# Attention that feeds a routed mixture of experts: the end flag read one double later and written after the slots, SyncE out of a barrier, the experts' first double in halves, and the first v load in five pieces with the queue held behind it

## The chip, the cores and the metric

The kernel runs on one core of a Trainium2 chip. The metric is the device time of one execution in microseconds (us). The engines are called as in the profile: PE is TensorE (matmuls), PEld its weight loads, DVE is VectorE, ACT is ScalarE, POOL is GpSimd, SP is SyncE. A `q` behind a name (PEldq, SPq) marks what that engine's sequencer does itself: register work, waits, branches, and the issue of DMAs.

## The reference

```python
scores = (1 / S) * z @ z.T              # 8 batches, S = 3072, z has 64 columns
attn   = maximum(scores, 0) ** 2
x      = (u * (attn @ v)).reshape(24576, 256)

logits = x @ w_gate                     # 8 experts, each token goes to its largest logit
gate_w = softmax probability of that expert
for i in range(24576):                  # in order: a token gets the next slot of its expert
    keep[i] = counts[e] < capacity      # capacity 768: later tokens of a full expert are dropped
h   = maximum(disp[e] @ w1[e], 0)       # 768 x 256 by 256 x 1024
y   = h @ w2[e]
out[i] = gate_w[i] * y[e, pos[i]]       # 0 for a dropped token
```

Tokens are placed in order, so once all eight experts are full no later token changes the output.

## The kernel before

The attention works through groups of 384 queries, eight groups to a batch, numbered n; g is n & 7. Group 0 is written out ahead of the loop ("peeled"). A group has twelve doubles c = 0..11, each of two chunks of 128 keys: four matmuls make scores into PSUM `Sc` (`scores`, L607 and L608), ACT applies Relu in place (L432) and squares into `attn` (L436), DVE splits the square into two fp16 parts (`attn_hi` L907, `attn_lo` L913), and 18 matmuls weigh v with them into `O` (`weigh`, L642, L644, L646). Scores run LEAD = 3 doubles ahead of the weighing; z and v are split into fp16 halves too (`first_z`, `v_hi`, `v_lo`), by scales from their maximum and their absolute sums (`v_sum`, L408, then DVE L925, a POOL reduction, three DVE steps).

At the end of group n-1 DVE multiplies `O` by u (`gate_x`, L952 and L956). During group n these rows are scaled and split (DVE L1005 writes the last part), SP transposes them by three DMAs (L259, `xT`), PE makes the logits at double 3 (L682), DVE picks the expert (L1041 to L1051), PE counts tokens (L690 to L697), and DVE works out the slots (L1067 to L1079). POOL scatters the rows to `disp` in HBM by three indirect DMAs (L350). In the same chain DVE writes a word to `ends` (L1074): 0 if all experts are full, NG + 1 otherwise. Every engine reads it in each group, after double END_AT (`load_end`, called by `both_parts`): it waits on `flag_ready`, loads the word into a register (L224), and branches. On 0, PE closes its accumulations (`close`, L708), issues filler matmuls that nobody reads (`turn_over`, L614), and leaves. The scores of double c + LEAD and their waits on the keys stand in the program ahead of the weighing of c; the matmuls for the norms of the next batch (`next_norms`, g = 3 alone) stand behind a branch at the end of double 6.

SP's part in group 0: load z and v of batch 0, `wg`, `ubuf`; fill the 6144 rows of `disp` with an empty row (eight DMAs from one SBUF row, L287); load z and v of batch 1 (L273, L278); wait until these have all landed (L216); and only then start on group 1, which begins with the three transposes. All of it is one queue, in program order. POOL waits for the fill (`disp_filled`) before it lets DVE overwrite rows.

The experts follow: five engines meet at `attention_over`, SP waits for PE (`pe_over`) and for the scatters, then loads dispatched rows by a transposing DMA and their tail (factor and token) by a plain one (`load_rows`, L315, L317). Per block of 384 rows there are four doubles of the hidden layer: 12 matmuls (`hidden`, L755), ACT Relu to fp16 (`high`, L541), DVE the rest (`low`, L1207). `hidden` of double q waits for `low` of double q - 2, since they share PSUM. DVE's factors come from the tails (`row_factors`, L1202).

## Time and profile before

| what | value |
|---|---|
| median of 3 runs | 886.45 us (885.63 to 886.87) |
| profiled execution, its own time | 889.07 us |
| its span | 887.3 us |
| PE busy, share of the span | 867.8 us, 98% |
| DVE, ACT, POOL busy | 71%, 64%, 14% |
| granted TensorE clock, mean | 0.996 |

The profiled execution took 2.6 us more than the median; the span is 1.8 us shorter than its own time. Busy time of PE counts pipelined matmuls whose ends are modelled, so a start-to-start distance says more of its pace than the busy share: 0.11 us for a matmul with 256 columns, 0.16 us for one with 384, at the full clock. The scored part of the loop ends at about 621 us, in group 18.

### The profile page before, as it was taken

Reading aid. Unit: us, or ns where it says so; the run is one execution under the profiler, and the core shown is the slowest. Engines: PE = TensorE matmul, PEld = TensorE weight load, DVE = VectorE, ACT = ScalarE, POOL = GpSimd, SP = SyncE. Lnnn points to the kernel's source line nnn. Section 1 sums busy time; section 2 is a strip of 40 time slices with the busy share of each in tenths; the row PEclk is TensorE's granted clock in tenths of the full one; section 3 lists DMA queues with packets and bytes.
Section 4 is the critical chain, followed back from the end, with each engine's and each line's share of the span. In section 5 each row is a group of like instructions: output and inputs, shape, how many; then the busy total and the mean of one; then the engine's idle time right before and its main releaser. Section 6 shows DMA issues by size and latency. Waiting matters only on the chain.

```text
span 887.3 us, 22840 instructions
## 1 busy us (share of the span) xinstructions
PE 867.8 (98%) x7397; PEld 690.7 (78%) x7398; DVE 630.9 (71%) x1346; ACT 572.1 (64%) x871; POOL 120.2 (14%) x119
## 2 busy tenths in 40 slices
PE   5999999999999999999999999999899999999997
PEld 4877787887788888888888888888677777777776
DVE  6976867888888888788888887677255565655531
ACT  6968776768768669787777876777144344434422
POOL 0001102101101101110110110110112112121212
PEclk8999999999999999999999999999999999999999
DMA  9955619624633650110111012411714245225100
GB/s 287 205 190 179 195 36 348 195 57 139 195 89 107 232 178 20 51 41 24 42 53 25 28 51 55 168 42 35 166 42 150 54 130 166 84 94 154 51 20 35
DMA packets 105991, 97.87 MB, mean 110 GB/s; under 512 B 63869, under 2 KB 94666, under 8 KB 104816
## 3 DMA queue, kind: packets, MB, share of 16 engines
q1 hardware_dynamic: 101072, 84.92, 32.9%
q0 software_dynamic: 4896, 12.64, 4.0%
q8 instruction: 14, 0.23, 0.1%
q14 instruction: 9, 0.07, 0.0%
HBM read 40.03 MB, written 44.93 MB: 96 GB/s over the span
## 4 chain that ended last, share of the span: by engine, by line
PE 91%; DMA 3%; issue 2%; ACT 1%; SPq 1%; DVE 1%; POOL 0%; ACTq 0%; POOLq 0%; DVEq 0%
PE O L642 16%; PE O L646 15%; PE O L644 15%; PE Sc L755 14%; PE Sc L607 8%; PE Sc L608 8%; PE O L776 3%; PE O L778 3%; PE O L780 3%; DMA rawv<-in_v 2%; PE M L778 2%; PE M L776 2%; PE M L780 2%; ACT Sc L432 1%; PE M L682 1%
## 5 line engine op out<-in xcount | busy, mean ns | idle before, releaser
L646 PE MATMUL O<-vS,attn_lo 128*128 128x256 f16 x1332 | 363.0, 273 | 0.0
L642 PE MATMUL O<-vS,attn_hi 128*128 128x256 f16 x1332 | 363.0, 273 | 0.0
L644 PE MATMUL O<-vS,attn_hi 128*128 128x256 f16 x1332 | 363.0, 273 | 0.0
L913 DVE TENSOR_TENSOR attn_lo<-attn,attn_hi 128x768 f16<-128x768 f32 x224 | 214.7, 958 | 7.7
L432 ACT ACTIVATE Sc<-Sc 128x768 f32<-128x768 f32 x224 | 178.2, 795 | 51.7 <-PE Sc L608 41.3
L436 ACT ACTIVATE attn<-Sc 128x768 f32<-128x768 f32 x224 | 181.7, 811 | 7.1
L607 PE MATMUL Sc<-zP 128*128 (+1 forms) x450 | 147.3, 328 | 7.0 <-ACT attn L436 5.3
L642 PEld LDWEIGHTS O<-vS,attn_hi 128*128 128x128 f16 x1332 | 130.3, 98 | 27.6 <-DVE ubuf L952 1.0
L644 PEld LDWEIGHTS O<-vS,attn_hi 128*128 128x128 f16 x1332 | 130.3, 98 | 26.5
L907 DVE CAST attn_hi<-attn 128x768 f16<-128x768 f32 x224 | 125.3, 560 | 34.1 <-ACT attn L436 30.3
L608 PE MATMUL Sc<-zQ,zP 128*128 (+1 forms) x450 | 147.0, 327 | 0.0
L1207 DVE SCALAR_TENSOR_TENSOR rawv<-Sc,rawv 128x768 f16<-128x768 f32 x64 | 61.1, 956 | 113.9 <-ACT rawv L541 113.9
L646 PEld LDWEIGHTS O<-vS,attn_lo 128*128 128x128 f16 x1332 | 130.3, 98 | 15.1
L350 POOL DMA_INDIRECT disp<-xrow,slot x54 | 68.6, 1270 | 480.3 <-DVE slot L1078 444.3
L541 ACT ACTIVATE rawv<-Sc 128x768 f16<-128x768 f32 x64 | 51.9, 811 | 114.5 <-PE Sc L755 113.2
L755 PE MATMUL Sc<-vS,w1h 128*128 128x384 f16 x512 | 104.1, 326 | 2.0 <-DVE rawv L1207 1.6
L755 PEld LDWEIGHTS Sc<-vS,w1h 128*128 128x128 f16 x512 | 49.9, 98 | 30.5 <-ACT rawv L541 1.9
L776 PE MATMUL O<-w2s,rawv 128*128 128x256 f16 x256 | 69.8, 273 | 0.0
L780 PE MATMUL O<-w2s,rawv 128*128 128x256 f16 x256 | 69.8, 273 | 0.0
L778 PE MATMUL O<-w2s,rawv 128*128 128x256 f16 x256 | 69.8, 273 | 0.0
L607 PEld LDWEIGHTS Sc<-zP 128*128 128x128 f16 (+1 forms) x450 | 44.0, 98 | 31.4 <-ACT attn L436 9.6
L385 POOL DMA_INDIRECT out<-attn,vS x48 | 46.9, 977 | 123.5 <-ACT attn L553 109.7
(147 smaller groups left out, 891.1 us busy)
## 6 DMA issues: line engine op xcount, KB each, us to landing
out<-empty SPq DMA_DIRECT2D x8, 3072.0 KB, 11.7
wraw<-in_moe_w SPq DMA_DIRECT2D x16, 1024.0 KB, 7.7
rawv<-in_v SPq DMA_DIRECT2D x12, 768.0 KB, 11.6
ubuf<-in_u SPq DMA_DIRECT2D x19, 384.0 KB, 3.2
disp<-empty SPq DMA_DIRECT2D x8, 774.0 KB, 17.8
rawz<-in_z SPq DMA_DIRECT2D x3, 768.0 KB, 6.3
rawv<-in_v SPq DMA_DIRECT2D x1, 1024.0 KB, 7.5
rawv<-in_v SPq DMA_DIRECT2D x1, 896.0 KB, 9.2
```

What stands on the lines that cost most here:

```text
L432: act.activation(pair, pair, ACT.Relu).then_inc(s["relu_done"], 1)
L436: act.activation(attn[:, c % BUFS, :, :], Sp[:, 2 * (c % 2):2 * (c % 2) + 2, 0:GROUP], ACT.Square, scale=ROOT_C).then_inc(s["square_done"], 1)
L607: nc.tensor.matmul(to, keys, zP[:, bass.ds(qb, GROUP)], start=True, stop=False)
L608: ins = nc.tensor.matmul(to, keys, zQ[:, bass.ds(qb, GROUP)], start=False, stop=True)
L642: nc.tensor.matmul(o_part(t), hi, v[:, 0:D], start=c == 0 and j == 0 and t % 2 == 0, stop=False, skip_group_check=True)
L644: nc.tensor.matmul(o_part(t), hi, v[:, D:2 * D], start=False, stop=False, skip_group_check=True)
L646: ins = nc.tensor.matmul(o_part(t), lo, v[:, 0:D], start=False, stop=c == PAIRS - 1 and j == 1, skip_group_check=True)
L755: ins = nc.tensor.matmul(Sp[:, 2 * (p % 2) + fi, 0:GROUP], w[par][:, m, f * P:(f + 1) * P], xt[:, k, x + m, :], start=(at == 0), stop=(at ...
L776: nc.tensor.matmul(y_part(t), hi, w2s[:, par, f, 0:D], start=f == 0, stop=False, skip_group_check=True)
L778: nc.tensor.matmul(y_part(t), hi, w2s[:, par, f, D:2 * D], start=False, stop=False, skip_group_check=True)
L907: dve.tensor_copy(attn_hi[:, b, :, :].rearrange("p j n -> p (j n)"), attn[:, b, :, :].rearrange("p j n -> p (j n)")).then_inc(s["hi_done"], 1)
L913: dve.tensor_tensor(attn_lo[:, b, :, :], attn[:, b, :, :], attn_hi[:, b, :, :], ALU.subtract).then_inc(s["lo_done"], 1)
```

## The change

Four parts, with fillers set anew around them. (1) END_AT goes from 5 to 6, and DVE computes the slots first and the flag behind them, with two more waits of its own steps. (2) SP no longer counts in `attention_over`: 3 instead of 4. (3) The first double of the experts: PE signals after the first of its two halves (`h_first`), ACT and DVE handle it in two halves, and DVE does the first two doubles ahead of the two `row_factors`. (4) v of batch 0 comes in pieces of 4, 6, 6, 5, 3 chunks instead of 8, 7, 5, 4, and SP waits for the last piece before it issues `wg` and all behind it. Fillers: 40 to 56 and 20 to 28 at the beginning, 72 to 44 after `close`, 56 to 36 after the barrier. In group 0 the scores of double 3 stand behind the weighing of double 0.

```diff
@@ SP, group 0
-            for q, name in enumerate("abcd"):
+            for q, name in enumerate("abcde"):
                 sp.dma_start(rawv[:, V0_PIECES[q]:V0_PIECES[q + 1], :], v[0, :, V0_PIECES[q]:V0_PIECES[q + 1], :]
                              ).then_inc(s["loaded_v0" + name], 16)
+            sp.wait_ge(s["loaded_v0e"], 16)
             sp.dma_start(wg[:, :, :], w_gate).then_inc(s["loaded_wg"], 16)
...
             attention_loop(sp, body)
-            sp.sem_inc(s["attention_over"], 1)
             sp.wait_ge(s["pe_over"], 1)
@@ ACT, experts
-            high(0, 0)
+            act.wait_ge(s["h_first"], 1)
+            act.activation(hh[:, 0, 0, :], Sp[:, 0, 0:GROUP], ACT.Relu).then_inc(s["hh_first"], 1)
+            act.wait_ge(s["h_ready"], 1)
+            act.activation(hh[:, 0, 1, :], Sp[:, 1, 0:GROUP], ACT.Relu).then_inc(s["hh_done"], 1)
             high(1, 1)
@@ PE
             scores(1, 0, 1, 0)
-            turn_over(40)
+            turn_over(56)
             scores(2, 0, 2, 0)
-            turn_over(20)
+            turn_over(28)
...
-                            scores(K0 + c + LEAD, n, c + LEAD, par)
+                            if not peeled or c:
+                                scores(K0 + c + LEAD, n, c + LEAD, par)
...
+                        if peeled and c == 0:
+                            scores(K0 + LEAD, n, LEAD, par)
...
-                    turn_over(72)
+                    turn_over(44)
...
-            pe.wait_ge(s["attention_over"], 4)
-            turn_over(56)
+            pe.wait_ge(s["attention_over"], 3)
+            turn_over(36)
...
+                    if isinstance(q, int) and q == 0 and fi == 0:
+                        ins.then_inc(s["h_first"], 1)
@@ DVE, slots
-                            dve.tensor_tensor(base[:, 1, :], base[:, 0, :], M[1][:, 32:32 + E], ALU.add)
                             route(dve.tensor_tensor(posf[:, :, :], counts, over_tiles(base[:, 0, :]), ALU.add))
-                            dve.tensor_tensor(over[:, :], base[:, 1, :], limit[:, :], ALU.subtract)
+                            dve.tensor_tensor(base[:, 1, :], base[:, 0, :], M[1][:, 32:32 + E], ALU.add)
                             route(dve.tensor_tensor(fullp[:, :, :], posf[:, :, :], over_tiles(limit[:, :]), ALU.is_ge))
-                            dve.tensor_reduce(least[:, :], over[:, :], AX.X, ALU.min)
                             route(dve.scalar_tensor_tensor(out=posf[:, :, :], in0=fullp[:, :, :], scalar=float(FAR // 2),
                                                            in1=posf[:, :, :], op0=ALU.mult, op1=ALU.add))
+                            route(dve.tensor_tensor(posf[:, :, :], posf[:, :, :], onehot[:, :, :], ALU.mult))
+                            dve.tensor_reduce(slot[:, :], posf[:, :, :], AX.X, ALU.max).then_inc(s["slot_ready"], 1)
+                            route(dve.tensor_tensor(over[:, :], base[:, 1, :], limit[:, :], ALU.subtract))
+                            route(dve.tensor_reduce(least[:, :], over[:, :], AX.X, ALU.min))
                             dve.tensor_scalar(ends[0:1, bass.ds((n - 1) & (NG - 1), 1)], least[0:1, :],
                                               0.0, float(NG + 1), ALU.is_lt, ALU.mult
                                               ).then_inc(s["flag_ready"], 1)
-                            route(dve.tensor_tensor(posf[:, :, :], posf[:, :, :], onehot[:, :, :], ALU.mult))
-                            dve.tensor_reduce(slot[:, :], posf[:, :, :], AX.X, ALU.max).then_inc(s["slot_ready"], 1)
@@ DVE, experts
+            for fi, done in enumerate(("hh_first", "hh_done")):
+                dve.wait_ge(s[done], 1)
+                ins = dve.scalar_tensor_tensor(out=hl[:, 0, fi, :], in0=Sp[:, fi, 0:GROUP], scalar=0.0,
+                                               in1=hh[:, 0, fi, :], op0=ALU.max, op1=ALU.subtract)
+            ins.then_inc(s["hl_done"], 1)
+            low(1, 1)
             row_factors(0, 0)
             row_factors(0, 1)
-            low(0, 0)
-            low(1, 1)
@@ constants
-V0_PIECES = (0, 8, 15, 20, 24)
+V0_PIECES = (0, 4, 10, 16, 21, 24)
-END_AT = 5
+END_AT = 6
```

Three places show what this does to the order on an engine. The first is SP's queue from its third row on, at the beginning of the program, before the change (`rawv` is v, `disp<-empty` the fill, the last two rows the load of batch 1).

```order
L242 DMA rawv<-in_v 128x2048
L242 DMA rawv<-in_v 128x1792
L242 DMA rawv<-in_v 128x1280
L242 DMA rawv<-in_v 128x1024
L244 DMA wg<-in_moe_w_gate 128x16
L260 DMA ubuf<-in_u 128x768
L287 DMA disp<-empty 128x6x258 [waits empty_ready]
L287 DMA disp<-empty 128x6x258 x7
L273 DMA rawz<-in_z 128x1536 [waits klo_ready,khi_ready]
```

The same stretch with the change; the fill, 6.2 MB, now stands behind a wait on v.

```order
L242 DMA rawv<-in_v 128x1024
L242 DMA rawv<-in_v 128x1536 x2
L242 DMA rawv<-in_v 128x1280
L242 DMA rawv<-in_v 128x768
L245 DMA wg<-in_moe_w_gate 128x16 [waits loaded_v0e]
L261 DMA ubuf<-in_u 128x768
L288 DMA disp<-empty 128x6x258 [waits empty_ready]
L288 DMA disp<-empty 128x6x258 x7
L274 DMA rawz<-in_z 128x1536 [waits klo_ready,khi_ready]
```

What moved is `wg`, `ubuf` and everything after them: they can't be issued before v has landed.

The second place is PE's read of the flag inside the loop, before the change: it stands between the last matmul of double 5 and the scores issued in double 6, which carry waits on the keys.

```order
L646 MATMUL O<-vS,attn_lo 128x256
L224 REGISTER_ALU [waits flag_ready]
L224 REGISTER_ALU
L224 ISA
L224 TENSOR_LOAD ends
L207 COMPARE_AND_BRANCH
L198 REGISTER_ALU x2
L601 REGISTER_ALU [waits khi_ready,klo_ready]
L607 MATMUL Sc<-zP 128x384 [waits square_done]
```

With the change it stands one double further down, behind the branch for the norms (its four matmuls are skipped unless g is 3).

```order
L207 REGISTER_ALU
L207 COMPARE_AND_BRANCH
L585 MATMUL M<-zsq,onesb 128x384 [waits norm_step]
L585 MATMUL M<-zsq,onesb 128x384 x3
L207 UNCONDITIONAL_BRANCH
L224 REGISTER_ALU [waits flag_ready]
L224 REGISTER_ALU
L224 ISA
L224 TENSOR_LOAD ends
L207 COMPARE_AND_BRANCH
L604 REGISTER_ALU
L610 MATMUL Sc<-zP 128x384 [waits square_done]
```

The key waits are no longer behind the read, and the norms' branch is now ahead of it.

The third place is DVE's tail of the slot chain with the change (before it, the flag's three instructions stood among those of the slots, as the diff shows).

```order
L1080 TENSOR_TENSOR posf<-posf,onehot 128x24
L978 REGISTER_ALU
L1081 TENSOR_REDUCE slot<-posf 128x3
L1082 TENSOR_TENSOR over<-base,limit 128x8
L978 REGISTER_ALU
L1083 TENSOR_REDUCE least<-over 128x1
L978 REGISTER_ALU
L1084 REGISTER_ALU
L1084 ISA
L1084 TENSOR_SCALAR ends<-least 1x1
L1087 COPY base<-base 128x8
L914 REGISTER_ALU
```

The slot is written before the flag is begun, and the next cast of `attn` stands behind both.

## Rows read from the trace of the kernel before

**Rows 1.** Who waited for whom, whole span: us in total, times, longest.
```profile
PE Sc L607 <- ACT attn L436: 5.3, 2, 5.0
...
DVE ends L1074 <- DVE posf L1072: 4.0, 18, 0.2
...
PE Sc L755 <- DVE rawv L1207: 1.6, 1, 1.6
...
PE M L682 <- DMA xT<-xrow: 0.6, 1, 0.6
```

**Rows 2.** Timeline of the beginning: start, us, engine line operation, idle before.
```profile
17.04 1.06 ACT L408 ACTIVATE vS<-rawv 128x1024 f16<-128x1024 f32 x1 [2.38 <-DMA rawv<-in_v]
...
18.22 0.80 ACT L432 ACTIVATE Sc<-Sc 128x768 f32<-128x768 f32 x1
...
19.91 0.50 PE L607 MATMUL Sc<-zP 128*128 128x384 f16 x1 [5.02 <-ACT attn L436]
...
21.36 1.01 DVE L896 SCALAR_TENSOR_TENSOR vS<-rawv,vscale,vS 128x768 f16<-128x768 f32 x1
...
24.35 0.27 PE L642 MATMUL O<-vS,attn_hi 128*128 128x256 f16 x1
```

**Rows 3.** Stretches: length; PE, PEld, DVE, ACT, POOL busy; PEclk, DMA share, GB/s.
```profile
0.00:14.00 14.00, 9.42 (x93) 8.12 (x95) 9.32 (x65) 7.68 (x10) 0.21 (x5) 1.00 0.86 315
...
16.00:18.00 2.00, 0.00 (x0) 0.00 (x0) 0.00 (x0) 0.96 (x1) 0.00 (x0) 0.82 1.15 217
...
20.00:24.00 4.00, 4.00 (x27) 2.99 (x28) 3.93 (x6) 3.94 (x6) 0.00 (x0) 0.50 1.10 218
...
44.00:52.00 8.00, 8.00 (x70) 6.60 (x68) 5.75 (x12) 4.97 (x7) 0.36 (x1) 1.00 1.01 382
```

**Rows 4.** Line L216, SP's sequencer behind its wait for batch 1: ns; start.
```profile
L216 SPq MOVE  x1: 29/29/29, 56.8 to 56.8; - x1
```

**Rows 5.** The critical chain from group 1's first transpose to its logits: start, us, what.
```profile
59.97 1.31 SPq L259
...
63.79 2.42 DMA xT<-xrow
...
66.35 0.45 PE M L682 x12
```

**Rows 6.** Loads of the flag (L224), groups 1 to 7, then 8 to 18: ns min/median/max, starts.
```profile
L224 PEldq TENSOR_LOAD <-ends x7: 895/932/1203, 70.8 to 266.0; - x7
...
L224 PEldq TENSOR_LOAD <-ends x11: 302/306/320, 298.6 to 619.7; - x11
```

**Rows 7.** PE's sequencer around the read in group 2, by line: ns; first and last start.
```profile
L200 PEldq EVENT_SEMAPHORE  x3: 51/51/51, 102.9 to 105.0; - x3
...
L198 PEldq ALU_OP  x2: 36/36/36, 104.6 to 104.7; - x2
...
L601 PEldq ALU_OP  x2: 32/32/32, 101.0 to 105.1; - x2
...
L207 PEldq ALU_OP  x1: 36/36/36, 105.9 to 105.9; - x1
L207 PEldq COMPARE_BRANCH  x1: 213/213/213, 106.0 to 106.0; - x1
```

**Rows 8.** Timeline, the gap on PE behind that read.
```profile
104.76 0.27 PE L646 MATMUL O<-vS,attn_lo 128*128 128x256 f16 x1
105.22 0.33 PE L607 MATMUL Sc<-zP 128*128 x1 [0.19 <-issue]
```

**Rows 9.** Timeline around the end of the attention loop.
```profile
621.55 4.18 PE L614 MATMUL O<-ones,identh 128*128 128x128 f16 x72
626.27 3.30 PE L614 MATMUL O<-ones,identh 128*128 128x128 f16 x56 [0.54 <-SPq L310]
```

**Rows 10.** Timeline of the experts' first doubles.
```profile
634.58 1.81 DVE L1207 SCALAR_TENSOR_TENSOR rawv<-Sc,rawv 128x768 f16<-128x768 f32 x2
...
635.67 0.81 PE L755 MATMUL Sc<-vS,w1h 128*128 128x384 f16 x4 [1.56 <-DVE rawv L1207]
```

More of the change, by code:

```diff
@@ L177, in y_part @@
             return (Oa[:, 0, 0:D], Mp[:, 0, 0:D], Oa[:, 1, 0:D])[t]
-        names = """consts empty_ready loaded_z00 loaded_z01 loaded_wg loaded_v0a loaded_v0b loaded_v0c loaded_v0d
+        names = """consts empty_ready loaded_z00 loaded_z01 loaded_wg loaded_v0a loaded_v0b loaded_v0c loaded_v0d loaded_v0e
             zsq0 v_high vparts0 vsum0 nrm0 mx0 amx0 scales0 vsum_done nrm_psum nrm_done zhi_ready khi_ready zlo_ready klo_ready loaded_zv loaded_u loaded_w0 loaded_w1
@@ L189, in relu2_attention_moe @@
             h_ready hh_done hl_done y_summed y_ready y_scattered0 y_scattered1 y_scattered2
-            y_scattered3 fac_ready"""
+            y_scattered3 fac_ready h_first hh_first"""
         s = {n: sem(n) for n in names.split()}
@@ L409, in v_sum @@
                                       ACT.Abs, scale=1.0 / SUM_SCALE, accum_out=vsum[:, bass.ds(column, 1)])
-            for q in range(SLICES):
-                act.wait_ge(s["loaded_v0" + "abcd"[q]], 16)
+            for q in range(len(V0_PIECES) - 1):
+                act.wait_ge(s["loaded_v0" + "abcde"[q]], 16)
                 v_sum(q, V0_PIECES[q], V0_PIECES[q + 1] - V0_PIECES[q]).then_inc(s["vparts0"], 1)
@@ L536, in _ @@
             act.sem_inc(s["y_ready"], TILES)
-            act.wait_ge(s["attention_over"], 4)
+            act.wait_ge(s["attention_over"], 3)
             def high(q, p):
@@ L923, in _ @@
             first_z(2)
-            dve.wait_ge(s["vparts0"], SLICES)
-            dve.tensor_reduce(mx[:, 1:2], vsum[:, 0:SLICES], AX.X, ALU.add).then_inc(s["vsum0"], 1)
+            dve.wait_ge(s["vparts0"], len(V0_PIECES) - 1)
+            dve.tensor_reduce(mx[:, 1:2], vsum[:, 0:len(V0_PIECES) - 1], AX.X, ALU.add).then_inc(s["vsum0"], 1)
             dve.wait_ge(s["amx0"], 1)
@@ L1066, in over_tiles @@
                                 return x.unsqueeze(1).to_broadcast([P, TILES, E])
+                            route(dve.tensor_tensor(posf[:, :, :], counts, over_tiles(base[:, 0, :]), ALU.add))
                             dve.tensor_tensor(base[:, 1, :], base[:, 0, :], M[1][:, 32:32 + E], ALU.add)
-                            route(dve.tensor_tensor(posf[:, :, :], counts, over_tiles(base[:, 0, :]), ALU.add))
-                            dve.tensor_tensor(over[:, :], base[:, 1, :], limit[:, :], ALU.subtract)
                             route(dve.tensor_tensor(fullp[:, :, :], posf[:, :, :], over_tiles(limit[:, :]), ALU.is_ge))
-                            dve.tensor_reduce(least[:, :], over[:, :], AX.X, ALU.min)
                             route(dve.scalar_tensor_tensor(out=posf[:, :, :], in0=fullp[:, :, :], scalar=float(FAR // 2),
                                                            in1=posf[:, :, :], op0=ALU.mult, op1=ALU.add))
+                            route(dve.tensor_tensor(posf[:, :, :], posf[:, :, :], onehot[:, :, :], ALU.mult))
+                            dve.tensor_reduce(slot[:, :], posf[:, :, :], AX.X, ALU.max).then_inc(s["slot_ready"], 1)
+                            route(dve.tensor_tensor(over[:, :], base[:, 1, :], limit[:, :], ALU.subtract))
+                            route(dve.tensor_reduce(least[:, :], over[:, :], AX.X, ALU.min))
                             dve.tensor_scalar(ends[0:1, bass.ds((n - 1) & (NG - 1), 1)], least[0:1, :],
@@ L1196, in _ @@
             dve.drain().then_inc(s["attention_over"], 1)
-            dve.wait_ge(s["attention_over"], 4)
+            dve.wait_ge(s["attention_over"], 3)
             def row_factors(i, k):
@@ L1268 @@
 VLO_AT = (7, 8)
-ROUTE_STEPS = 2 + 2 + 2 + 4 + 3
+ROUTE_STEPS = 2 + 2 + 2 + 3 + 6
 _INS = ['u', 'v', 'z', 'moe_w_gate', 'moe_w1', 'moe_w2']
```

## The prediction, as put on record before the changed kernel ran

> **What bounds the kernel now.** I read four views: who waited for whom over the span, the timeline of the beginning, the critical chain, and the timeline around the end of the attention loop. PE is the engine that sets the end. It is busy 98% of the span, and nearly all its waits after its start stand in five places. In the waits view the reader is to see how short that list is: 5.0 us once at the beginning, where PE waits for ACT's first squares; 1.6 us once in the experts; 0.6 us once for a transpose [rows 1]; 0.5 us once for SP [rows 9]. A fifth kind is small and repeated, a gap where PE's sequencer issued nothing in time: in group 2 the last matmul of double 5 starts at 104.76 and the next at 105.22, 0.46 apart where 0.11 is due, so 0.35 us are lost [rows 8]. So an edit is worth what it takes from these places, less what it makes late elsewhere. The profiled execution took 889.07 us, 2.6 more than the median of 886.45; all terms are differences within the trace, and I take them over to the median unchanged. About 0.2%, 1.8 us, is what a measurement of this kernel can tell from no change.
>
> **1. The flag read, six gaps of 0.35 us and one larger.** The sequencer reaches the wait for the flag at 102.9 and the first scores behind it start at 105.22, so its path is 2.3 us long [rows 7, 8]. It runs ahead of the array by what is queued: the last queued matmul gives out at 104.87, 1.95 us after 102.92. The longest piece of the path is the load of the flag, 0.93 us in groups 1 to 7, 0.31 later [rows 6]; at 0.31 the path is 1.7 and fits in 1.95, so the gap is a matter of groups 1 to 7. With the change the pieces from the first L198 at 104.6 to L601 at 105.1 (key waits, 0.5 us) fall out of the path, and the norms' branch comes ahead of the wait: L207 at 105.9, then a branch of 0.213 from 106.0, some 0.37 in all [rows 7]. The path becomes 2.3 - 0.5 + 0.37 = 2.15, the gap 0.2 instead of 0.35: 0.15 in each of six groups, and about 0.25 in group 1, where the load took 1.2. Sum -1.2 us. Bounds: 0, if the branch and the load cost more behind the norms, and 6 x 0.35 + 0.7 = -2.8, if no gap is left. I take -1.2, worked out from the pieces. That the flag is written a little later (behind the slots) costs nothing: the read moves by a whole double, 2.6 us. DVE's cast behind the slots is delayed by two waits of its own steps, some 0.2 us each as the flag's wait now [rows 1], under the 2.6 us of a double by which the splits run ahead of PE.
>
> **2. The end of the loop, one double more.** The double adds 4 x 0.16 + 18 x 0.11 = 2.6 us on PE and 28 fillers of 0.058 fall away, -1.6. The fillers ended at 621.55 + 4.18 = 625.73, and SP let PE go on at 626.2, so SP was last by 0.5 [rows 9]. Now PE's drain comes at 625.73 + 1.0 = 626.7, and SP, which waits for it too, is ready before: the slots lose the flag's instructions ahead of them, whose last alone made DVE wait 0.2, 18 times [rows 1]. The rows of the experts are asked for 0.5 later. That SP is out of the barrier is therefore worth nothing: PE frees itself, but the rows set the start. +0.5 us; bounds 0 (drain earlier than modelled) and +1.0.
>
> **3. The first double in halves.** PE stood idle for 1.56 us until 635.67, when DVE's first `low` came in, which started only at 634.58 behind two factor steps that wait for tails [rows 10]. With `low` ahead of them and halves of 0.45 to 0.55 us on ACT and DVE, the first double is split at about 3 us after PE starts, PE needs 3.9 for its two doubles, and the wait is gone: -1.7, the idle 1.56 and the tail of a matmul that the idle time leaves out. Bounds: -1.7 and -1.0, the latter, if the second double's `low`, queued behind on DVE and needed 3.9 later, or the row loads come into it.
>
> **4. The beginning.** Two things happen. First, v lands earlier. ACT waited 2.38 us for the last piece, until 17.04, so it could have started at 14.66 [rows 2]; the landing is between these, and I take 15.6, the middle, since nothing but v is then in the queue. ACT then has 3 chunks instead of 4 (-0.2), so Relu starts 1.3 before its 18.22. PE's first weighing needs the first split of v, which ended at 22.37; it started at 24.35 for want of PE [rows 2]. At the full clock PE would be there at 21.1, and the moved scores (0.65) follow: a gain G of 24.35 - 21.1 - 0.65 = 2.6 us. At half clock, which was granted from 17.3 (0.82 of 2 us from 16 on) to 24 in and after PE's idle 5 us [rows 3], scores and 28 fillers take 1.3 + 3.0 us from 18.6, so 22.9 and G = 0.3 to 0.8. Fillers of 56 leave 2.8 us of idle, not 5, so both are open. Either way PE is up to 2.6 us early in group 0.
>
> Second, the fill of `disp` starts later, and group 1 hangs on it. Before, 14 us at 315 GB/s moved 4.4 MB [rows 3]; z, v, `wg` and `ubuf` are 4.3 MB, so the fill began by 13.9. Now `wg` is issued at 15.6, `ubuf` at 16.1, the fill at 16.6; with 1.1 us to the first byte, as for z at the start, and 1.1 us for `ubuf`, the fill flows from 18.35. That is 4.45 us later. The DMA share is 1.0 or more from there to 52, at 217 GB/s in the fill and 382 in batch 1 [rows 3], so nothing absorbs the delay. SP's wait for batch 1 ended at 56.8, three microseconds before the rows of group 1 were there to be transposed at 59.97, so it cost nothing [rows 4, 5]. It now ends at 56.8 + (3.9 to 4.6) = 60.7 to 61.4, and the transposes start 0.3 later, at 61.0 to 61.7 instead of 59.97. From the first issue to the last landing they took 6.24 us (59.97 to 63.79 + 2.42) [rows 5]; back to back, two issues of 1.31 and the last one's 2.42 are 5.0 at least. The logits, at 66.35 before, come at 66.1 to 68.0. PE would have been there at 65.5 - G. So the gain of the beginning is waited away in group 1, and this term is 0 to +1.6; I take +0.5. What hid the fill was ACT's and DVE's work in group 0; what is late next is `xT`. Past it, everything on PE follows the logits as before.
>
> Against this the Trainium skill speaks (DMA: Bandwidth & Descriptors, Rules for kernel authors and Specifications): issue a DMA early and wait late, and the fabric carries up to 435 GB/s with rows above 512 bytes at line rate. The first half is against the new wait. By the second, an estimate, the fill of 6.2 MB would take 14 us and batch 1 would be in long before 57, and term 4 would be -G. The rows of the fill are 1032 bytes and ran at half that rate, so the sum goes by the trace.
>
> **Sum.** -1.2 + 0.5 - 1.7 + 0.5 = -1.9 us: 884.5.
>
> **Rivals.**
> A, the forecast: the terms above, 883.2 to 886.0.
> B, the queue is in time: the fill catches up, or L216 ends by 59, and PE keeps G. For it: ACT's 2.38 us wait for the last piece of v, while the fill is already flowing at the same time [rows 2, 3], says that some part of the DMA engines runs behind the others; if the end of batch 1 is theirs too, they lose less by the hold than the others do. Against it: a DMA share over 1.0, that is no slack in the mean. Then -2.4 - (1.0 to 2.6) = 881.4 to 883.0.
> C, slower than before: PE waits 2.5 to 3.5 us at the logits of group 1, and the clock is halved for it, as it was after 5.0 us of idle and was not after 1.6 in the experts [rows 1, 3]: the mean clock of 0.996 leaves room for one half-clock stretch of 7 us in the span, and that is the one at the beginning. A stretch at half clock is 6.7 us long in the trace (17.3 to 24) and loses half of that, 3.4: 884.5 + 3.4 = 887.9, and 889 if v lands as late as before (+1.4). It decides from a wait of some 2.5 us on, so it needs both a G near 2.6 and the late fill. The Trainium skill (TensorE: Matmul & The Clock Gate, Part 1) has the throttled clock as the default that activity lifts, which the trace bears out at the start; it gives no other time here.
> D, the read does not gain: term 1 is 0, since the branch for the norms takes what the key waits give. 885.7.
>
> **How the numbers follow.** A 0.47, B 0.25, C 0.20, D 0.08. Below 884.7 lie B and about half of A: faster 0.50. Within 0.2% lie the rest of A, D and half of C: 0.40. Slower 0.10. The range takes in B down to 881.8 and C up to 887.8.
>
> **What would show it.** Term 1: the gap behind L224's load in groups 2 to 7 at 0.2, no L198 between load and scores. Term 2: PE's drain near 626.7, less what came before, and SP's first expert load right behind it. Term 3: no wait of L755 for `rawv`. Term 4: SPq L216 at 60.7 or later instead of 56.8; L682 waiting for `xT` 1.5 to 4 us; first weighing at 21 or 22.9. Wrong if L216 stays near 57 to 58 (B), or if PEclk shows 0.5 in group 1 (C).

## The result, and the profile after

The changed kernel took 892.34 us (median of 4 runs, 891.41 to 893.28) against 886.12 us (4 runs) for the kernel before: ratio 1.0065, interval 1.005 to 1.008. It is slower; 884.5 was forecast, with 887.8 as the upper end. The profiled execution took 893.28 us with a span of 891.5.

First, who waited on PE over the whole span (total, times, longest), the view of [rows 1]:

```profile
PE M L686 <- DMA xT<-xrow: 5.9, 2, 5.0
...
PE Sc L610 <- ACT attn L436: 3.6, 4, 1.2
PE Sc L761 <- DMA vS<-disp: 1.3, 1, 1.3
```

The wait for ACT's first squares (5.0 in [rows 1]) is short now, and the wait for DVE's `low` in the experts is gone. In their place PE waits 5.0 us, once, for the transposed rows `xT` ahead of the logits of group 1. The stretches around it (length; PE, PEld, DVE, ACT, POOL busy; PEclk, DMA share, GB/s) and the logits themselves, as in [rows 3, 5]:

```profile
62.00:67.60 5.60, 0.61 (x15) 0.36 (x14) 0.00 (x0) 0.00 (x0) 0.00 (x0) 1.00 0.42 81
67.70:71.00 3.30, 3.30 (x17) 2.01 (x15) 1.80 (x11) 2.29 (x4) 0.00 (x0) 0.50 0.91 319
71.10:76.00 4.90, 4.90 (x48) 4.01 (x47) 3.89 (x14) 3.40 (x6) 1.91 (x2) 1.00 1.03 349
...
67.30 0.45 PE L686 MATMUL M<-wgs,xT 128*128 128x16 f16 x12 [4.99 <-DMA xT<-xrow]
```

All engines stand still for it, and the 3.3 us behind it run at half clock: 1.7 us lost. SP's wait for batch 1, the fill of `disp` and the batch's first load show why, against 56.8 in [rows 4]:

```profile
15.61 19.41 SPq L288 DMA_DIRECT2D disp<-empty  x8
35.13 4.67 SPq L274 DMA_DIRECT2D rawz<-in_z  x1
...
L216 SPq MOVE  x1: 29/29/29, 61.4 to 61.4; - x1
```

The beginning of PE did what was hoped, and more (compare [rows 2]; at 24.35 before):

```profile
16.95 0.34 PE L610 MATMUL Sc<-zP 128*128 128x384 f16 x1 [1.16 <-ACT attn L436]
...
19.66 0.27 PE L645 MATMUL O<-vS,attn_hi 128*128 128x256 f16 x1 [0.33 <-DVE vS L904]
```

Behind group 1 the changed kernel loses more. In groups 2, 9 and 10 there is a wait for ACT's square in the second half of the group (start, us, idle time before), where [rows 1] had one such wait beside that of the beginning, 0.3 us in group 9:

```profile
120.92 0.27 PE L649 MATMUL O<-vS,attn_lo 128*128 128x256 f16 x1
121.91 0.33 PE L610 MATMUL Sc<-zP 128*128 x1 [0.72 <-ACT attn L436]
...
350.08 0.33 PE L610 MATMUL Sc<-zP 128*128 x1 [1.11 <-ACT attn L436]
...
381.95 0.27 PE L649 MATMUL O<-vS,attn_lo 128*128 128x256 f16 x1
382.87 0.33 PE L610 MATMUL Sc<-zP 128*128 x1 [0.64 <-ACT attn L436]
```

A yardstick for the loop is the time from group 1's logits to group 18's. These are the last ones, before and after, with the first hidden matmul of the experts behind them (the starts are what counts here; of the logits' twelve matmuls the rows hold only those in the stretch that was asked for):

```profile
615.40 0.25 PE L682 MATMUL M<-wgs,xT 128*128 128x16 f16 x4
630.04 0.82 PE L755 MATMUL Sc<-vS,w1h 128*128 128x384 f16 x4 [0.47 <-DMA vS<-disp]
```

```profile
620.88 0.17 PE L686 MATMUL M<-wgs,xT 128*128 128x16 f16 x1
...
635.96 0.82 PE L761 MATMUL Sc<-vS,w1h 128*128 128x384 f16 x4 [1.27 <-DMA vS<-disp]
```

So the loop takes 615.40 - 66.35 = 549.05 us before and 620.88 - 67.30 = 553.58 after, of which 1.7 is the half clock; the loop's end takes 14.64 and 15.08.

### The profile page after: what moved, and what is told of

Same layout as the page of the kernel before. It is cut to its first block, busy times and chain, and to the rows that moved or that the text cites. A ratio compares the mean times of both kernels' runs of the same rounds, so it can differ in the third digit from the quotient of the medians.

```text
span 891.5 us, 22911 instructions
## 1 busy us (share of the span) xinstructions
PE 868.9 (97%) x7395; PEld 690.5 (77%) x7396; DVE 634.7 (71%) x1349; ACT 573.8 (64%) x878; POOL 114.4 (13%) x119
## 4 chain that ended last, share of the span: by engine, by line
PE 80%; DVE 6%; issue 5%; ACT 3%; DMA 3%; ACTq 1%; SPq 1%; PEld 1%; DVEq 0%; POOL 0%; PEldq 0%; POOLq 0%
PE Sc L761 14%; PE O L645 13%; PE O L647 13%; PE O L649 13%; PE Sc L610 7%; PE Sc L611 6%; PE O L784 3%; PE O L786 3%; PE O L788 3%; DMA rawv<-in_v 2%; ACT Sc L432 2%; PE M L786 2%; PE M L784 2%; PE M L788 2%; DVE attn_hi L915 1%
## 5 line engine op out<-in xcount | busy, mean ns | idle before, releaser
L432 ACT ACTIVATE Sc<-Sc 128x768 f32<-128x768 f32 x225 | 179.1, 796 | 55.6 <-PE Sc L611 46.5
L350 POOL DMA_INDIRECT disp<-xrow,slot x54 | 62.4, 1156 | 490.0 <-DVE slot L1081 449.5
```

The lines of the kernel that those rows point to most:

```text
L432: act.activation(pair, pair, ACT.Relu).then_inc(s["relu_done"], 1)
```

## The experiments

Four series on four chips; each comparison is with the kernel before on the same chip, in the same series. "Loop" below is the yardstick just named, read from each run's own trace.

### What the hold costs: no_hold

```diff
-            sp.wait_ge(s["loaded_v0e"], 16)
             sp.dma_start(wg[:, :, :], w_gate)...
```

> The changed kernel without SP's wait for the last piece of v; all else stays. Theory (the hold makes batch 1 late, PE waits 5 us for xT in group 1 and is then granted half the clock for 3.4 us): L216 ends near 57, the wait for xT in group 1 falls under 1 us, PEclk stays at 1.00 from 62 to 76, and all groups from group 2 on start 2.6 us earlier than in the changed kernel: 889.7 us, and down to 888.5 if PE also keeps part of what it gained in group 0. Rival (the half clock in group 1 comes from the longer fillers and the moved scores, not from the wait): PEclk still falls in group 1 and the time stays at 891 or more. Second rival (v lands later again without the hold and eats what is won): the first weighing starts at 24 instead of 19.7, but since group 1's logits set the pace, 889.7 stays.

886.44 us, ratio 1.0002 (0.9992 to 1.0012). L216 ended at 52.9, and group 1's logits waited for nothing of note:

```profile
61.71 0.45 PE L685 MATMUL M<-wgs,xT 128*128 128x16 f16 x12
```

The clock stays at 1.00, and the first weighing is at 19.9 without the hold too, so the second rival is out, and so is the first. The time came out 2 to 3 us under the 888.5 to 889.7 that were expected: the expectation went from 892.3, and what a slow fill does to the changed kernel is not in this series (see after_again). The forecast's B, an early group 1, is what this edit gives. But the loop takes 551.99, so 2.9 us are still lost in it, and v needs no hold to come early.

### ACT's read: act_read and both

Behind double 6 ACT first reads the flag, then sums v; `both` has no hold either.

```diff
                 def part(start, stop):
+                    if start and not peeled:
+                        extras(END_AT)
                     for c in range(start, stop):
...
-                        if not peeled and (c in VHI_AT or c in ZHI_AT):
+                        if not peeled and c != END_AT:
+                            extras(c)
```

> The changed kernel, with ACT's reading of the flag moved ahead of its own extra work of double 6 (the sum of v and the wait for it in groups 1, 2, 9, 10, 17 and 18); the hold of the fill stays. Theory (ACT's read is exposed behind the sum of v, where ACT's queue has been emptied, and costs 0.3 to 0.8 us each in groups 2, 9, 10 and 17): the gaps on PE of 0.88 in group 2, 1.27 in group 9, 0.80 in group 10 and 0.31 in group 17 go back to the 0.2 to 0.45 of their neighbours, and the time falls by 2 to 2.6: 890.0 us. Rival (those groups are late because DVE writes the flag and the slots later, or because of PE's own read): the gaps stay, 892.3. The 2.6 us of group 1 stay in both.

> The changed kernel without the hold and with ACT's read of the flag ahead of its extra work. Theory: the two costs are separate and add up, 892.3 - 2.6 - 2.3 = 887.4 us; what is left against the kernel before are the double more at the loop's end (+0.4), the halves in the experts (-1.7), PE's shorter gap behind the read (-0.7) and some 0.9 to 1.5 of groups 8 and 9 that neither names; without those, 884.5. Rival (they hide each other: with one gone, the other's delay is what remains): within 1 us of the better one of the two single edits.

act_read 886.98 (1.0014, 1.0003 to 1.0025), both 885.99 (0.9997, 0.9986 to 1.0008). The first number looks like a triumph of the theory (892.3 to 890.0 was expected) and is none: the time came from group 1, which this edit doesn't touch, and where the logits came at 62.73 instead of 67.30. Group 10 of the changed kernel, and then of act_read, on ACT:

```profile
370.26 0.19 ACT L408 ACTIVATION_READ_ACCUMULATOR xT<-rawv  x1
371.59 0.80 ACT L432 ACTIVATE Sc<-Sc 128x768 f32<-128x768 f32 x1 [1.14 <-issue]
372.42 0.81 ACT L436 ACTIVATE attn<-Sc 128x768 f32<-128x768 f32 x1
...
375.36 0.81 ACT L436 ACTIVATE attn<-Sc 128x768 f32<-128x768 f32 x1
```

```profile
363.42 0.84 ACT L408 ACTIVATE xT<-rawv 128x768 f16 x1 [0.80 <-issue]
364.17 0.19 ACT L408 ACTIVATION_READ_ACCUMULATOR xT<-rawv  x1
364.70 0.80 ACT L432 ACTIVATE Sc<-Sc 128x768 f32<-128x768 f32 x1 [0.34 <-ACT xT L408]
...
375.98 0.33 PE L616 MATMUL Sc<-zP 128*128 x1 [0.53 <-ACT attn L436]
```

1.14 us of idle behind the sum became 0.80 ahead of it and 0.34 behind it: the same. PE's wait in group 10 stayed (0.53 against 0.64), in group 2 (0.72) and in group 9 (1.01 against 1.11) as well. The edit moved the cost, it did not take it away, and couldn't tell the theory from its rival. `both` shows the same: loop 551.75 against 551.99 without the edit, 0.2 us, and a time within 0.5 us of no_hold's, as the rival had it.

### The changed kernel again, and the hold alone: after_again, hold_only

hold_only is the kernel before with one line more:

```diff
+            sp.wait_ge(s["loaded_v0d"], 16)
             sp.dma_start(wg[:, :, :], w_gate)...
```

> The changed kernel once more, with a profile, in one series with the others. In its first profile the fill of disp was issued from 15.6 on, batch 1 was in at 61.5 and PE waited 5.0 us for xT; with ACT's read moved (which should not touch group 1 at all) the fill was issued at 15.1, batch 1 was in at 56.9 and the wait was 0.9. Theory (the hold leaves batch 1 without slack, and the rate at which the fill and the batch run, which differs from execution to execution, then decides over 4 to 5 us): the time spreads over 886.5 to 893 over series, and the profile's wait for xT goes with the end of L216, 1.0 + (L216's end - 57) us. Rival (the moved read did it): 892 and a wait of 5.0 us again.

> The kernel before, with SP waiting for the last piece of v ahead of wg, ubuf and the fill, and nothing else. Theory (the hold brings v in earlier but batch 1 later): the first weighing at 21 to 22, L216's end 3 to 4 us later than the 53.9 to 56.8 seen without a hold, the logits of group 1 from 1 us earlier to 2 us later than before, 885.7 to 888.5; I put 886.7. Rival (the fill catches up, the hold costs nothing and v's gain stays): 884.

The changed kernel took 888.06 here, ratio 1.0028 (1.0016 to 1.004), not 1.0065. In its trace the fill, the batch and the logits:

```profile
15.02 16.97 SPq L288 DMA_DIRECT2D disp<-empty  x8
32.09 3.90 SPq L274 DMA_DIRECT2D rawz<-in_z  x1
...
L216 SPq MOVE  x1: 29/29/29, 57.0 to 57.0; - x1
...
62.82 0.44 PE L686 MATMUL M<-wgs,xT 128*128 128x16 f16 x12 [0.85 <-DMA xT<-xrow]
```

The issues of the fill, which stand in the queue behind the transfers, took 17.0 us instead of 19.4, the batch was in at 57.0 instead of 61.4, and PE waited 0.85 instead of 4.99; the theory, not the moved read. The loop takes 552.75. hold_only took 885.87, ratio 1.0001 (0.9991 to 1.0012): L216 ended at 55.6, the logits came at 64.00. Without a hold, before's beginning gives 62.27 to 63.52 in six traces (below), 62.27 in the one of this chip. So by the traces the hold alone makes group 1 late by 0.5 to 1.7 us with the fill at this speed; by the times it costs a microsecond at most, and they can't tell it from nothing.

### The dose: hold_mid and hold_more

```diff
             sp.wait_ge(s["loaded_v0e"], 16)
+            sp.wait_ge(s["vparts0"], len(V0_PIECES) - 1)
...
+            sp.wait_ge(s["v_high"], 1)
```

The first of the two lines is hold_mid, the second, in its place, hold_more.

> The changed kernel with SP held about 1.5 us longer ahead of wg, ubuf and the fill (until ACT has summed the last piece of v). In the second series L216 ended at 57.0 and PE waited 0.9 us for xT. Theory (the end of L216 moves with the hold, and PE's wait with it): L216 at 58.4, the wait at 2.3 us, 888.1 + 1.4 = 889.5. By the forecast's case C the clock halves from a wait of some 2.5 us on, so it is open here: with it, 891. Rival (the fill and the batch catch up): L216 at 57, 888.

> The changed kernel with SP held some 4 us longer (until ACT has made the first split of v). Theory (the first measurement of the changed kernel was only one with a slower fill: L216 at 61.5, a wait for xT of 5.0, the clock at 0.5 for 3.4 us): L216 at 61, the wait at 4.9 us, the granted clock at 0.5 in group 1, 888.1 + 4.0 + 1.7 = 893.8. Rival (the halved clock was that execution's own and doesn't follow from the wait): 892.1, with the clock at 1.00.

hold_more took 893.52, ratio 1.0067 (1.0049 to 1.0084): the time of the changed kernel's first measurement, made at will by a longer hold. hold_mid took 888.7, ratio 1.0015 (1.0002 to 1.0027). The stretch behind the wait in hold_mid, then in hold_more:

```profile
63.93 0.44 PE L687 MATMUL M<-wgs,xT 128*128 128x16 f16 x12 [2.16 <-DMA xT<-xrow]
...
64.50:67.80 3.30, 3.30 (x16) 2.11 (x14) 1.72 (x11) 2.44 (x4) 0.00 (x0) 0.50 0.92 325
```

```profile
67.81 0.47 PE L687 MATMUL M<-wgs,xT 128*128 128x16 f16 x12 [5.38 <-DMA xT<-xrow]
...
65.70:72.40 6.70, 4.59 (x36) 3.13 (x37) 1.90 (x12) 3.13 (x5) 0.00 (x0) 0.50 0.76 234
```

The last column counts the executions whose granted clock, meant over the span, was under 0.999.

| | L216 ends | wait for `xT` | clock behind it | us | under 0.999 |
|---|---|---|---|---|---|
| no_hold | 52.9 | none | 1.00 | 886.44 | 0 of 11 |
| after_again | 57.0 | 0.85 | 1.00 | 888.06 | 1 of 8 |
| hold_mid | 58.1 | 2.16 | 0.50 for 3.3 us | 888.7 | 3 of 12 |
| changed kernel, first | 61.4 | 4.99 | 0.50 for 3.3 us | 892.34 | 4 of 4 |
| hold_more | 62.0 | 5.38 | 0.50 for 6.7 us, 2.1 of them still in the wait | 893.52 | 6 of 6 |

The wait follows L216's end, and the halved clock follows the wait. hold_mid stands on the edge: its profiled execution (889.91) is one of the three with a lower clock, which took 889.9 on average, the other nine 888.3. That is 1.6 us for the half clock, where the trace says 1.7, and it is why the median, taken over mostly undisturbed executions, is no further over before (2.05) than after_again's (2.08).

### Part 1: flag, slots, end_late

`flag` is the kernel before with part 1, `slots` with the new order of slots and flag alone, `end_late` with the later read alone:

```diff
-END_AT = 5
+END_AT = 6
...
-                    turn_over(72)
+                    turn_over(44)
```

These two edits are in flag and end_late; flag and slots have the reordered slots of the change's own diff.

> The kernel before with part 1 alone: slots ahead of the flag, the flag read a double later, 44 fillers instead of 72 at the end. In the runs that have part 1, groups 2, 3, 9, 10 and 17 each take 0.2 to 0.8 us more than in the kernel with the halves alone; those are the groups in which ACT sums v in doubles 6 to 9. Theory (ACT's read, in the double in which the sums begin, costs ACT 0.8 us in these groups, whether ahead of the sum or behind it; the other groups gain 0.1 each): +2.3 in the loop and +0.4 at its end, 888.4 to 888.8 against 885.7 to 886.1. Rival (the delays are the beginning's, which brings PE earlier to groups 1 and 2): at most +0.5 in the loop, 886.5. The forecast's own account: 885.4.

> The kernel before with the slots written ahead of the flag, and the flag still read at double 5. Theory (with the read left where it was, only the flag's 0.4 us of lateness counts; the cost of part 1 is the read's meeting with the first sum of v in double 6): 885.7 to 887.0, with gaps behind the read of 0.5 to 0.8 instead of 0.35 in every group, and no larger ones in groups 2, 9 and 10 than elsewhere. Rival (the order of the slots is what costs groups 2, 9 and 10): 888, with their gaps of 0.8 to 1.3.

> The kernel before with the flag read a double later (and 44 fillers instead of 72), the flag still written ahead of the slots. Theory (the read itself, in the double of the first sum of v, costs ACT 0.8 us in groups 1, 2, 9, 10, 17 and 18): PE's gaps behind the read go to 0.2 in most groups, but 0.75 in group 2, 1.2 in 9, 0.7 in 10, as in the run with part 1 whole; 1.4 us more than before, the same as part 1 whole. Rival (the slots' order is what costs): the gaps of groups 2, 9 and 10 are as small as the others', and the kernel is 0.5 to 1 us faster than before.

flag 887.42, ratio 1.0018 (1.0008 to 1.0028), loop 551.27, between the rival's 886.5 and the theory's 888.4. Its loop and the loop's end are 2.2 to 2.7 longer by the traces, and the time only 1.4: from the first double of the experts to the third it took 4.41 us where before took 5.63. PE's wait for `low` fell to 0.34 by itself there, a gain that isn't to be had beside the halves, which end that wait anyway. slots 895.92, ratio 1.0092 (1.0074 to 1.0111), loop 558.56. end_late 886.84, ratio 1.0011 (1.0001 to 1.0021), loop 551.80. In end_late the flag is written as early as before, and still:

```profile
115.58 0.27 PE L646 MATMUL O<-vS,attn_lo 128*128 128x256 f16 x1
116.44 0.33 PE L607 MATMUL Sc<-zP 128*128 x1 [0.59 <-ACT attn L436]
...
376.32 0.27 PE L646 MATMUL O<-vS,attn_lo 128*128 128x256 f16 x1
377.07 0.33 PE L607 MATMUL Sc<-zP 128*128 x1 [0.47 <-ACT attn L436]
```

The wait in group 9 is there too, 0.95. So the read's new place is enough to cost in groups 2, 9 and 10, with the old order of the slots. slots missed its expectation badly, by my arithmetic: gaps of 0.5 to 0.8 instead of 0.35 were expected "in every group", they came at 0.83, and that alone, times six, is 3 us, not the 1 us I put; on top of it the later groups lost 0.2 to 1.4 each, groups 9 and 10 most. There PE waits for ACT's square as well (1.09 and 0.62) though the read is at double 5: the flag comes so late that ACT's read is no longer under its own square (0.48 us of idle behind it in group 10). A late flag and a later read seem to end in the same wait; no run here takes them apart in these two groups. With the new order the read had to go to double 6; with the old order it had not.

### The sums moved away from the read: sum_late

The changed kernel without the hold, and:

```diff
-SUM_AT = (6, 7, 8, 9)
+SUM_AT = (7, 8, 9, 10)
```

> The changed kernel without the hold, and with ACT's four sums of v in doubles 7 to 10 instead of 6 to 9, so that the flag's read and the first sum lie in different doubles again. Theory (it is their meeting in double 6 that costs): the gaps on PE of 0.88, 1.29 and 0.80 us in groups 2, 9 and 10 go back to 0.2 to 0.5, the loop takes about 2 us less, 884.2 us. Rival (the sums are late anyway, and in double 10 they meet the squares of z or the logits of the next group): the gaps move to the end of the same groups, 886.4 or more.

884.82, ratio 0.9993 (0.9982 to 1.0004). The loop takes 550.12, 1.9 less than in no_hold, 0.8 and 0.7 of it in groups 1 and 2. Group 2's gap:

```profile
116.38 0.27 PE L648 MATMUL O<-vS,attn_lo 128*128 128x256 f16 x1
116.81 0.33 PE L609 MATMUL Sc<-zP 128*128 x1 [0.16 <-issue]
```

No wait for ACT is left there, and the theory that the read and the first sum cost by meeting holds in groups 1 and 2. The rival has a part: in groups 9 and 10, where the sums now run into the last doubles' other work, gaps of 1.3 and 0.6 us remained, the first as long as in no_hold. The median is 1.2 under before's, and the ratio can't be told from 1.

### The parts that don't cost: chunks, chunks_again, bar, chunks_begin, chunks_begin_bar

`chunks` is before with part 3, `bar` with SP out of the barrier, `chunks_begin` with part 3 and part 4 without its hold, `chunks_begin_bar` adds the barrier to that. The lines are those of the change; of part 3 and of the barrier:

```diff
+            act.wait_ge(s["h_first"], 1)
+            act.activation(hh[:, 0, 0, :], Sp[:, 0, 0:GROUP], ACT.Relu).then_inc(s["hh_first"], 1)
...
-            sp.sem_inc(s["attention_over"], 1)
-            act.wait_ge(s["attention_over"], 4)
+            act.wait_ge(s["attention_over"], 3)
```

> The kernel before with the experts' first double in halves and low ahead of the factor steps, and nothing else. Theory: PE's wait of 1.56 us ahead of the first output goes and nothing behind it becomes late: 886.1 - 1.7 = 884.4 us. Rival (the factor steps or the second double's low come late and take it back): 885.3 to 886.1, with a new wait of PE within the first four doubles of the experts.

> The kernel with the halves in the experts alone, once more, for comparison within this series: 0.998 of before, 1.7 us in the profile behind the first output.

> The kernel before with SP out of the barrier behind the loop. The forecast's theory (PE frees itself, but the rows that SP then loads set the start of the experts): no change, the first hidden matmul within 0.2 us of where it is without, counted from the last group. Rival (SP was last by 0.5 us, and that is saved): 0.4 to 0.5 us earlier, under what the times can tell but not under what the trace can.

> The kernel before with the halves in the experts and the beginning (v in five parts, 56 and 28 fillers, the third double's scores behind the first weighing), but no hold, no change of the flag and none at the loop's end. Theory (in the runs without the hold group 1's logits came 1.3 to 1.8 us earlier than in the kernel with the halves alone, and nothing behind takes it back when the flag is left where it was): 884.5 - 1.5 = 883.0 us. Rival (what is gained in group 0 is waited away in group 1, or in group 8 for xT): 884.5.

> The parts of the change that were not found to cost: the halves in the experts, the beginning without the hold, SP out of the barrier; the flag and its read are left as before. Theory: 1.5 to 2 us under the kernel with the halves alone (chunks_again), 3 us and a ratio of 0.9965 against before. Rival (what the beginning wins in the profile is only the straggler that an execution of either kernel has or has not): level with chunks_again, 0.998.

| | us | ratio | g1 logits | loop | loop end |
|---|---|---|---|---|---|
| chunks | 884.5 | 0.9981 (0.997 to 0.9991) | 63.52 | 549.40 | 14.52 |
| chunks_again | 884.19 | 0.9987 (0.9978 to 0.9996) | 62.95 | 549.40 | 14.44 |
| bar | 885.7 | 1.0003 (0.9992 to 1.0013) | 63.45 | 549.06 | 14.51 |
| chunks_begin | 885.61 | 0.9994 (0.9981 to 1.0007) | 62.08 | 549.03 | 16.74 |
| chunks_begin_bar | 886.23 | 1.0005 (0.9994 to 1.0015) | 62.01 | 549.12 | 16.21 |

The halves are the one part that pays, twice: DVE's two halves run as soon as ACT's are done, and the second double's `low` is ready in time. In chunks:

```profile
629.29 0.56 DVE L1218 SCALAR_TENSOR_TENSOR rawv<-Sc,rawv 128x384 f16<-128x384 f32 x1 [9.28 <-ACT rawv L557]
630.12 0.56 DVE L1218 SCALAR_TENSOR_TENSOR rawv<-Sc,rawv 128x384 f16<-128x384 f32 x1 [0.28 <-ACT rawv L559]
```

`bar` left the loop's end where it was, as the forecast had it. The beginning without the hold brought group 1's logits forward by 0.9 to 1.5 us against chunks and chunks_again (0.2 against flag, the earliest of before's beginnings) and kept that through the loop, and then lost it all at the loop's end: the first rows of the experts, asked for at 621.99 in chunks_begin, kept PE waiting until 627.86, where chunks_again asked at 623.24 and began at 626.80.

```profile
627.86 0.82 PE L761 MATMUL Sc<-vS,w1h 128*128 128x384 f16 x4 [2.50 <-DMA vS<-disp]
```

Both kernels of this kind show it, the changed kernel does not (asked at 632.33, begun at 635.96). In chunks_begin the first transfer of rows landed 5.8 us behind its issue, in chunks_again 3.5. Why those rows took 2.3 us longer I have not settled. And it isn't all: the profiled execution of chunks_begin_bar (884.64) is 1.6 under its median. Five of its eleven executions were granted a clock of 0.999 or more and took 884.7 on average, six were granted less and took 886.7; where those six lost their clock no trace shows. chunks_begin missed its 883.0 and came out level with chunks, as its rival had it (1.0 under before, against 1.2 and 1.5). chunks_begin_bar missed both its theory and its rival: it ended 2 us over chunks_again. The kernel with the halves alone is the best one here, 0.13 to 0.19% under before.

## Why the prediction was wrong

**Two steps failed: term 1 had the wrong sign, and term 4 was sized by a profiled execution that was not like the others.** Forecast was -1.9, measured +6.2. In the two profiled executions the terms add up: 67.30 - 66.35 = 0.95 for group 1's logits, 1.7 for the half clock behind them, 2.8 for the loop, 0.4 for its end, -1.7 for the halves, together 4.2, and 893.28 - 889.07 is 4.2. Against the forecast that is 4.0 more in the loop (term 1 stood at -1.2) and 2.2 more in term 4 (0.95 + 1.7 instead of 0.5). The last 2.0 lie in the step "I take them over to the median unchanged": before's profiled execution was 2.95 over its median of 886.12, after's 0.94 over its own.

**Term 4: the wait at group 1 was too small in the sum, the half clock was left to a rival, and the baseline was late.** SP's wait was to end at 60.7 to 61.4 and ended at 61.4, with the fill at 215 GB/s as in the profile before; in after_again, at 249 GB/s, it ended at 57.0, which the forecast had named as the sign of B. So the second half of the term, the late fill, was right for one speed of the fill and not for the other. The first half, what PE gains in group 0, was too small: v was in at 13.7, where 15.6 was taken, and the first weighing stood at 19.66, where 21.1 was the best case. The profile of before misled here. In it ACT waited until 17.04 for the last piece of v [rows 2]; in chunks, which loads v in the same way, until 14.55:

```profile
14.55 1.06 ACT L408 ACTIVATE vS<-rawv 128x1024 f16<-128x1024 f32 x1 [0.36 <-DMA rawv<-in_v]
```

The first weighing there stood 2.9 us earlier. The late piece also came with a longer half clock at the beginning: 6.7 us in before, 3.3 in chunks, bar, slots and end_late, none in flag and chunks_again. The granted clock of the whole span says how common that is. Of the 121 executions of before in the four series, 41 were granted 0.999 or more and took 884.9 on average, 61 were granted 0.997 or 0.998 (886.2), and 19 at most 0.996 (888.5); the profiled one, at 0.996 and 889.07, is of the last kind. Against an ordinary execution the five parts gain 0.2 to 1.5 (chunks_begin and chunks_begin_bar against flag and chunks), not 2.6. The logits were put at 66.1 to 68.0 and came at 67.30, but an ordinary execution of before has them at 62.27 to 63.52, not at 66.35 (flag, chunks_again, end_late, slots, bar and chunks, which are before up to there). The earliest and the latest of the six, flag and chunks:

```profile
62.27 0.17 PE L682 MATMUL M<-wgs,xT 128*128 128x16 f16 x1
```

```profile
63.52 0.17 PE L685 MATMUL M<-wgs,xT 128*128 128x16 f16 x1 [0.67 <-DMA xT<-xrow]
```

The wait was 5.0, over the 2.5 to 3.5 of C, and the clock was halved for 3.3 us, not 6.7: 1.7 lost instead of 3.4. So the term was put at +0.5 and is 67.30 - 62.3 or 63.5 + 1.7, +5.5 to +6.7, with the slow fill, and -0.7 to +0.6 (62.82) with the fast one. The hold by itself, against no_hold, is 5.6 and 1.7 in the one and 1.1 in the other. Rival C, a wait that halves the clock, was the right case for the first measurement. I gave it 0.20 because it needed "both a G near 2.6 and the late fill", from a limit of 2.5 us that I had put between the 1.6 and the 5.0 of the rows; hold_mid shows that 2.2 us of waiting can suffice, by the granted clock in 3 of 12 executions.

On the fill: the profile had 217 GB/s for rows of 1032 bytes, and the sum went by it. The Trainium skill's advice to issue a transfer early and wait late (DMA: Bandwidth & Descriptors, Rules for kernel authors) is borne out by no_hold. The estimate of 14 us for the fill, made from the 435 GB/s of the same page (Specifications), is not: the fill's issues alone took 17.0 to 19.4 us.

**Term 1 failed in sign.** It costed the gap behind PE's own read and found -1.2. The gap did shrink, from 0.35 to some 0.23 in groups 3 to 7, a gain of about 0.6. What was left out is the other reader. "The read moves by a whole double" was looked at for PE and for DVE's flag, not for ACT, whose read in double 5 lay under its own square and in double 6 meets the sum of v. In groups 1, 2, 9, 10, 17 and 18 ACT needs more for a double than PE does (square to square 372.42 to 375.36, 2.9 us, against 2.6), so up to 0.8 us there reach PE. Shown by end_late (the read alone: loop 551.80 against 549.05 to 549.40 with the read at double 5, 0.5 to 0.8 of it from a wait for `xT` in group 8) and by sum_late (read and sum apart: 550.12), for groups 1 and 2; the wait in group 9 stayed in sum_late, where the sums meet other work of ACT. Part 1 as a whole: loop 551.27, +1.9 to +2.2 where -1.2 was forecast.

**Term 2 was right**: +0.44 (14.64 to 15.08) for +0.5, and SP's leaving worth nothing (bar).

**Term 3 was right**: -1.7. From the first hidden matmul of the first double to that of the third it was 1.72 shorter, and the ratio of chunks says 0.1 to 0.3%.

The sum by the traces against ordinary executions, with the slow fill: 5.5 to 6.7 for the beginning and the hold, 2.8 for the loop (553.58 - 1.7 against 549.05), 0.4 for its end, -1.7 for the halves: +7.0 to +8.2, where the interval of the ratio is 4.4 to 7.1 and the medians differ by 6.2. The baseline of the first piece is from series whose fill was faster, which may be the excess. With the fast fill (after_again): -0.7 to +0.6, 3.4 to 3.7 for the loop (552.75), 0.4, -1.7: +1.4 to +3.0, and the medians differ by 2.1. Of those loops 1.9 to 2.2 are part 1; some 0.7 in the first trace is a wait for `xT` in group 8 (the second of the two in its waits), and of the remaining 1.5 in the second I know only that PE waited 1.2 us in all, three times, for `issue`, 0.5 of it in group 1, where before has such a wait too. What made the other two, in groups 9 and 17, I haven't found.

## What to carry to other kernels

When a read of a shared flag is moved, cost it on every engine that reads it: where it was free it lay under that engine's own work, and the same instruction a double later can meet the one place where that engine is behind. When a queue is held back, take the transfer that is needed first behind it and ask how much slack it had in several executions, not in one: against no_hold the same wait made the batch 4.1 us late in one trace here, at a cost of 1.1, and 8.5 us late in another, at a cost of 7.3, by the speed of the fill and by whether the wait was long enough to cost the clock too. And before differences are taken over to the median, look for what made the profiled execution slower than it, its granted clock first; that piece may be the very thing that the change removes.

## What the runs showed of the hardware

The same queue of transfers ran at different speeds in different series: the eight issues of the fill took 19.4 us in the first trace and 17.0 in the second of one and the same kernel. From 20 to 32 us, nearly all of it fill, the DMA engines moved 215 GB/s in the profiles of before and after, and 238 to 260 in all sixteen profiles of the four series. Whether the chip makes the difference isn't shown. And the last piece of v released ACT at 17.04 in one trace and 14.55 in another.

Executions of one kernel fall into groups by the granted clock. In before, the ones that had lost no more than 0.1% of it took 884.9 us on average, the ones at 0.997 or 0.998 886.2, the ones at 0.996 or less 888.5; half-clock stretches behind the first 10 us and ahead of the last 10 lasted 3.3 or 6.7 us in the traces.

A wait does not halve the clock by its length alone: 2.16 us ahead of group 1's logits were followed by 0.50 (hold_mid, its profiled execution), 2.50 us ahead of the experts were not (chunks_begin, the stretch behind the wait):

```profile
628.00:634.00 6.00, 6.00 (x39) 3.69 (x38) 2.31 (x5) 1.87 (x4) 0.00 (x0) 1.00 1.06 175
```

And the half clock lasted 3.3 us in two traces, with PE busy throughout, and 6.7 in a third, where it fell 2.1 us before PE had anything to do again.
